# Turning the tails of two score tiles with one transpose, and regrouping the value products, in an attention and two-layer kernel

## What is computed

```python
def _attn_ref(q, k, v, tau):
    scale = 1.0 / np.sqrt(q.shape[-1])
    scores = scale * np.matmul(q, k.transpose(0, 1, 3, 2))
    thresh = np.max(scores, axis=-1, keepdims=True) - tau
    scores = np.where(scores >= thresh, scores, -1000000000.0)
    scores = scores - np.max(scores, axis=-1, keepdims=True)
    attn = np.exp(scores)
    attn = attn / (np.sum(attn, axis=-1, keepdims=True) + 1e-09)
    return np.matmul(attn, v)
# layer 1: h = x @ w_in (512 x 2048), g = h * tanh(softplus(h)), x = g @ w_out
# layer 2: h = x @ w_in, g = h * clip(h + 3, 0, 6) / 6, out = g @ w_out
```

## Time and profile before

| | |
|---|---|
| median of 3 runs | 1047.8 us (1047.51 to 1048.72) |
| the profiled execution | 1048.76 us |
| its span, first to last instruction | 1046.6 us |
| attention, first row maximum to that of the last pair | 9.0 to 300.8 us |
| PE busy over the span | 1024.9 us (98%) |
| DVE, ACT, POOL busy | 855.6, 662.0, 546.7 us |

### The profile page before, as it was taken

How to read it: one execution, slowest core, us unless ns; L and a number is a source line. 1 busy time by engine, 2 the same in 40 slices (tenths; PEclk the granted TensorE clock), 3 DMA queues, 4 the chain that set the end, 5 groups by cost and what they waited for, 6 DMA issues and landing times.

```text
span 1046.6 us, 19806 instructions
## 1 busy us (share of the span) xinstructions
PE 1024.9 (98%) x6856; PEld 920.5 (88%) x6856; DVE 855.6 (82%) x1694; ACT 662.0 (63%) x1241; POOL 546.7 (52%) x562
## 2 busy tenths in 40 slices
PE   6999999999999999999999999999999999999998
PEld 5666666666666999999999999999999999999998
DVE  7877877877773889978997889967996779968884
ACT  6778777778885566555664566646564655655643
POOL 7787887888983770078204770087103760068200
PEclk9999999999999999999999999999999999999999
DMA  6364564564542799869895899742785448843674
GB/s 189 103 215 144 161 215 143 162 215 140 177 146 82 225 327 308 321 199 294 297 371 187 266 328 315 289 142 106 250 310 163 165 164 274 281 151 127 221 242 161
DMA packets 136034, 224.37 MB, mean 214 GB/s; under 512 B 9216, under 2 KB 76288, under 8 KB 135936
## 3 DMA queue, kind: packets, MB, share of 16 engines
q1 hardware_dynamic: 135936, 223.12, 64.4%
HBM read 172.49 MB, written 50.59 MB: 213 GB/s over the span
## 4 chain that ended last, share of the span: by engine, by line
PE 79%; DVE 8%; ACT 7%; issue 4%; DMA 1%; SPq 0%; DVEq 0%; ACTq 0%
PE banks L601 8%; PE banks L548 7%; PE banks L666 7%; PE banks L668 7%; PE banks L667 7%; PE banks L703 6%; PE banks L702 6%; PE banks L701 6%; PE banks L709 5%; PE banks L711 5%; PE banks L710 5%; PE banks L560 5%; PE banks L556 3%; ACT relu L870 3%; PE banks L581 2%
## 5 line engine op out<-in xcount | busy, mean ns | idle before, releaser
L1330 POOL TENSOR_TENSOR ring<-raw,ring 128x256 fp32r<-128x256 f32 x336 | 282.3, 874 | 379.5 <-ACT ring L835 379.5
L666 PE MATMUL banks<-x_high,ring 128*128 128x384 f32 x672 | 226.7, 337 | 1.5 <-ACT probsT L774 0.8
L668 PE MATMUL banks<-x_high,ring 128*128 128x384 f32 x672 | 224.8, 334 | 0.0
L667 PE MATMUL banks<-x_low,ring 128*128 128x384 f32 x672 | 224.6, 334 | 0.0
L1010 DVE TENSOR_REDUCE neg_max<-banks 128x1 f32<-128x576 f32 x144 | 108.0, 750 | 55.6 <-PE banks L548 55.2
L703 PE MATMUL banks<-ring,g_low 128*128 128x256 f32 x504 | 142.6, 283 | 0.0
L702 PE MATMUL banks<-ring,g_high 128*128 128x256 f32 x504 | 142.6, 283 | 0.0
L701 PE MATMUL banks<-ring,g_high 128*128 128x256 f32 x504 | 142.6, 283 | 0.0
L666 PEld LDWEIGHTS banks<-x_high,ring 128*128 128x128 f32 x672 | 126.1, 188 | 7.7 <-issue 4.9
L667 PEld LDWEIGHTS banks<-x_low,ring 128*128 128x128 f32 x672 | 126.2, 188 | 0.0
L668 PEld LDWEIGHTS banks<-x_high,ring 128*128 128x128 f32 x672 | 126.1, 188 | 0.0
(11 more groups left out here) (100 smaller groups left out, 2227.7 us busy)
## 6 DMA issues: line engine op xcount, KB each, us to landing
ring<-w_out_mix SPq DMA_DIRECT2D x168, 512.0 KB, 5.0
raw<-w_in_mix SPq DMA_DIRECT2D x48, 896.0 KB, 5.9
w_in_mix<-prep_in SPq DMA_DIRECT2D x18, 896.0 KB, 5.4
w_out_mix<-prep_high SPq DMA_DIRECT2D x16, 896.0 KB, 4.7
w_out_mix<-prep_low SPq DMA_DIRECT2D x16, 896.0 KB, 5.8
q_raw<-qT SPq DMA_DIRECT2D x64, 144.0 KB, 2.9
k_raw<-kT SPq DMA_DIRECT2D x64, 144.0 KB, 2.9
prep_in<-w_in SPq DMA_DIRECT2D x64, 128.0 KB, 3.3
```

The source lines that it names most:

```text
L666: nc.tensor.matmul(dst, w[:, 0, cols], high, start=(t == 0 and m < 4), stop=False, skip_group_check=True)
L667: nc.tensor.matmul(dst, w[:, 0, cols], low, start=False, stop=False, skip_group_check=True)
L668: mm = nc.tensor.matmul(dst, w[:, 1, cols], high, start=False, stop=(t == KH - 1), skip_group_check=True)
L1330: nc.gpsimd.tensor_tensor(ring_slot(slot)[:, 1, :], raw[q % 2][:, m, :], f32(ring_slot(slot)[:, 0, :]), ALU.subtract).then_inc(w_low_ready, 1)
```

## The change

It has four parts.

1. **Tails.** The keys are put in another column order. An even tile of a pair holds keys 320 to 575, 0 to 255, and then the tail (now keys 256 to 319). An odd tile holds the tail first. The two stand next to each other in `probs`, so one 128 x 128 transpose turns both tails. Only tiles 1, 3, 5, 7 and 8 turn a tail (five per pair in place of nine), and ACT copies 128 x 128 into a new tile `tailT` (`TURNS` = 5 places). The half of the rows that belongs to the other tile meets zeros in a new tile `values_tail`, so these products have 128 rows in place of 64, and go in blocks of 128 query columns (one of 64), head after head. A tile's scores are now 320 and 256 columns, written side by side across a bank boundary. Values come in four transfers per pair in place of two.
2. **Value products** stand in four tiles (4, 6, 8, and 1 of the pair after) in place of seven. These steps turn an even tile or, at step 1, tile 8.
3. **Weight rounding** in four pieces (512, 512, 512, 256 columns), after steps 15, 16, 17 and 1. The split follows in four pieces too, and so do the late units during the layers.
4. `spread_sums` takes 128 rows everywhere.

```diff
-    PART_AT = (0, MAIN // 2 * P, SEQ)
+    X_KEYS = MAIN // 2 * P
+    Y_KEYS = X_KEYS + TAIL
+    TURNS = MAIN + 1
+    def tails_turned(t):
+        return t // PAIR_TILES * TURNS + t % PAIR_TILES // 2
+    def tail_first(i):
+        return i % 2 == 1
+    def turns_tail(i):
+        return tail_first(i) or i == PAIR_TILES - 1
+    def key_ranges(i):
+        return ((X_KEYS, SEQ), (0, X_KEYS)) if tail_first(i) else ((Y_KEYS, SEQ), (0, Y_KEYS))
...
-        scores = [banks[:, 2 * s:2 * s + 2, 0:HALF] for s in range(3)]
+        def scores_at(s):
+            first, last = key_ranges(s % PAIR_TILES)[0]
+            return BANK - (last - first)
+        def scores_of(s):
+            return bank_pair(s)[:, scores_at(s):scores_at(s) + SEQ]
+        def probs_of(t):
+            at = SEQ if tail_first(t % PAIR_TILES) else 0
+            return probs[:, tails_turned(t) % 2, at:at + SEQ]
...
-        PREP_PARTS = (slice(0, 4), slice(4, MIXES))
+        PREP_PARTS = (slice(0, 2), slice(2, 4), slice(4, 6), slice(6, MIXES))
...
-                        after(pe, tail_kept, t - 2)
+                        after(pe, tail_kept, tails_turned(max(t - 2, 0)))
...
-                nc.tensor.transpose(turned_tail[s % 3], probs[:, s % 3, SEQ - P:SEQ], ident[:, :]).then_inc(tail_turned, 1)
+                i, own = t % PAIR_TILES, probs_of(t)
+                if turns_tail(i):
+                    tail = probs[:, tails_turned(t) % 2, SEQ - TAIL:SEQ + TAIL] if tail_first(i) else own[:, SEQ - P:SEQ]
+                    nc.tensor.transpose(turned_tail[s % 3], tail, ident[:, :]).then_inc(tail_turned, 1)
...
-                    rows = slice(0 if j < MAIN else P - TAIL, P)
                     for a in range(2):
-                        mm = nc.tensor.matmul(mixed[u][DH * a:DH * a + DH, :], values[rows, b, j, DH * a:DH * a + DH],
-                                              probsT[b][rows, a, j, PART_AT[u]:PART_AT[u + 1]], start=(j == 0), stop=(j == MAIN))
+                        if j < MAIN:
+                            nc.tensor.matmul(mixed[u][DH * a:DH * a + DH, :], values[:, b, j, DH * a:DH * a + DH],
+                                             probsT[b][:, a, j, PART_AT[u]:PART_AT[u + 1]], start=(j == 0), stop=False,
+                                             skip_group_check=True)
+                            continue
+                        for c0 in range(PART_AT[u], PART_AT[u + 1], P):
+                            i = a * (MAIN + 1) + c0 // P if c0 < MAIN * P else MAIN
+                            first, n = (0, P) if i != MAIN else (TAIL * a, TAIL)
+                            rows = tail_rows(i)
+                            mm = nc.tensor.matmul(mixed[u][DH * a:DH * a + DH, c0 - PART_AT[u]:c0 - PART_AT[u] + n],
+                                                  values_tail[:, b, rows, DH * a:DH * a + DH],
+                                                  tailT[:, b, i // 2, first:first + n], start=False, stop=True, skip_group_check=True)
...
-            part0 = {4: (0,), 5: (1, 2), 6: (3, 4)}
-            part1 = {7: (0, 1), 8: (2,), 0: (3,), 1: (4,)}
+            part0 = {4: (0, 1), 6: (2, 3, 4)}
+            part1 = {8: (0, 1, 2), 1: (3, 4)}
...
-                act.wait_ge(tail_turned, t + 1)
+                if turns_tail(i):
+                    act.wait_ge(tail_turned, tails_turned(t) + 1)
+                    nc.scalar.copy(tailT[:, p, i // 2, :], turned_tail[s % 3]).then_inc(tail_kept, 1)
...
-                    if s == 16 and it < ITS - 1:
-                        round_prep(0, it, 0)
+                    if s in (15, 16, 17) and it < ITS - 1:
+                        round_prep(0, it, s - 15)
                     if s == 1 and it > 0:
-                        round_prep(0, it - 1, 1)
+                        round_prep(0, it - 1, 3)
```

More of the change, by code:

```diff
@@ L9 @@
 F32R = mybir.dt.float32r
-AX_XY = mybir.AxisListType.XY
+AX_X = mybir.AxisListType.X
 P = 128
@@ L544, in score_tile @@
                     if half == 1:
-                        after(pe, tail_kept, t - 2)
+                        after(pe, tail_kept, tails_turned(max(t - 2, 0)))
+                    first, last = key_ranges(i)[half]
+                    begin = BANK if half else scores_at(s)
                     for n, (lhs, rhs) in enumerate(products):
-                        mm = nc.tensor.matmul(scores[s % 3][:, half, :], lhs, rhs[:, HALF * half:HALF * (half + 1)],
+                        mm = nc.tensor.matmul(bank_pair(s)[:, begin:begin + last - first], lhs, rhs[:, first:last],
                                               start=(n == 0), stop=(n == len(products) - 1))
@@ L581, in spread_sums @@
                             mm = nc.tensor.matmul(mixed[u][DH * a:DH * a + DH, c0 - PART_AT[u]:c1 - PART_AT[u]],
[L582 to L583 removed]
+                                                  recips[:, b, col:col + 1].to_broadcast([P, DH]),
+                                                  ident[:, first + c0 - P * i:first + c1 - P * i], start=True, stop=True)
                 mm.then_inc(spread_ready, 1)
@@ L622, in attention_step @@
                         mix(it, pair, b, 0, part0[i])
-                    if i in (7, 8):
+                    if i == 8:
                         mix(it, pair, b, 1, part1[i])
-                if not first and i in (0, 1):
+                if not first and i == 1:
                     mix(it, pair - 1, 1 - b, 1, part1[i])
@@ L745, in round_k, with keep_main @@
                 nc.scalar.copy(k_high[k][:, :], k_raw[k % 2][:, :]).then_inc(k_high_ready[k], 1)
-            def keep_main(t, s):
+            def keep_main(t, s, pair):
                 p, i = s // PAIR_TILES, s % PAIR_TILES
                 act.wait_ge(main_turned, t + 1)
+                if i == 0:
+                    after(act, mixed_ready, 2 * pair - 2)
                 if i == MAIN:
@@ L792, in attention_step, with round_prep @@
                     after(act, probs_ready, t - 1)
-                    nc.scalar.activation(halves(exps[:, s % 2, :]), scores[s % 3], ACT.Exp,
+                    nc.scalar.activation(exps[:, s % 2, :], scores_of(s), ACT.Exp,
                                          bias=neg_max[:, s % 3:s % 3 + 1], scale=1.0).then_inc(exp_ready, 1)
                 if (not first or s >= 2) and (ahead or s < 2):
-                    keep_main(t - 2, (s - 2) % TILES_IT)
+                    keep_main(t - 2, (s - 2) % TILES_IT, it * PAIRS_IT + (s - 2) // PAIR_TILES)
                 if ahead and s in rounds:
                     round_k(it, rounds[s])
-            def round_prep(layer, u, half):
+            def round_prep(layer, u, n):
                 unit = QUADS * layer + u
@@ L939, in _ @@
                     if unit < LATE_UNITS and part == 1:
-                        for half in range(2):
-                            round_prep(*late_unit(unit), half)
+                        for n in range(len(PREP_PARTS)):
+                            round_prep(*late_unit(unit), n)
                     for b in (B22, B11, B12):
@@ L1145, in rest_prep @@
             def rest_prep(layer, u):
-                for half, mixes in enumerate(PREP_PARTS):
-                    dve.wait_ge(prep_out_rounded, 2 * (QUADS * layer + u) + half + 1)
+                for n, mixes in enumerate(PREP_PARTS):
+                    dve.wait_ge(prep_out_rounded, len(PREP_PARTS) * (QUADS * layer + u) + n + 1)
                     nc.vector.tensor_tensor(prep_low[:, mixes, :], prep_out[:, mixes, :], f32(prep_high[:, mixes, :]),
@@ L1302, in rest_prep @@
             def rest_prep(u):
-                for half, mixes in enumerate(PREP_PARTS):
-                    pool.wait_ge(prep_out_rounded, 2 * u + half + 1)
+                for n, mixes in enumerate(PREP_PARTS):
+                    pool.wait_ge(prep_out_rounded, len(PREP_PARTS) * u + n + 1)
                     nc.gpsimd.tensor_tensor(prep_low[:, mixes, :], prep_out[:, mixes, :], f32(prep_high[:, mixes, :]),
```

76 lines of the change are left out of this document (39 added, 37 removed).

## The result

| | before | after |
|---|---|---|
| median (runs) | 1047.72 us (4) | 1040.88 us (4, 1039.96 to 1042.2) |
| ratio | | 0.9936, 95% interval 0.9922 to 0.995 |
| span of the profiled execution | 1046.6 us | 1038.1 us |
| middle pair (mean of ten) | 19.61 us | 18.78 us |
| last row maximum | 318.6 us | 304.3 us |

The change makes the kernel 6.8 us faster, 0.64%. The forecast was 17.3. (The last maximum of before is at 318.6 us; the 300.8 in the table ahead is where the last pair begins.) The times between two row maxima come from the starts of that instruction, nine to a pair. The first products of the layers come in rounds of eight units, and the last row of the table is the time from the first product of a round's first unit to that of its eighth, in the second and the third round.

A forecast was written before the change was run, and what follows sets the result against it. PE's own sequence was taken to bound the attention. A gain of 1.2 us per middle pair (-12.0 for ten), smaller gains in other pairs and 0.4 given back made -17.3 us: 1030.5 us forecast, range 1026 to 1041.

The forecast's parts named there:

- The layers do not change: Layers after the attention: PE back to back, no change expected; a change above 2 us would show the prediction wrong.
- Tail transposes, -0.44: PE in attention: four tail transposes fewer per pair at 0.109 us each, -0.44 us.
- The wait behind the tail copy: Scores held behind ACT's tail copy, itself behind a rounding: 0.53 us per iteration, expected to go.
- Three groups at 0.30, -0.90: PE in attention: seven groups of value products become four, three saved at 0.30 us, -0.90 us per pair.
- Tail products, +0.06 side by side or +0.71: PE's tail products per pair: +0.06 us if both heads run at once, +0.71 us if one follows the other.
- Spread, -0.10: PE's spread of sums: 64 columns of 128 rows replace the 64-row end, -0.10 us per pair taken.
- The walk: Nine tiles stepped through three engine queues: 18.2 us per changed pair, 18.85 if heads run one after the other.
- Waits: PE's waits per pair in attention: 0.6 us before, about 0.75 us forecast after, from uneven tiles.
- DVE and ACT can't catch up: Rival, attention tiles: DVE's 1.52 us per tile holds PE, +1.9 us per pair, 1075 us; chance 0.04 (slower).
- The four-piece rounding does not do its part: Rival: POOL falls behind and delays heads, 1 to 3 us off the gain; inside the range, no separate chance.
- Heads one after the other: Rival, tail products: the second head waits for the first, 0.65 us per pair, 9 us, 1039.5 us; chance 0.33.
- No wait is left: Rival, attention: PE's work alone sets the time, -2.15 us per pair, 1018 us; chance 0.04.

The follow-up runs named there:

- e1: The changed kernel with weight rounding and splitting back in two pieces everywhere: 1035.14 us, ratio 0.9872.
- e2: The changed kernel with four rounding pieces for units rounded during the attention and two for the late units in the layers: 1035.84 us, ratio 0.9882.
- e7: The changed kernel, but in the layers ScalarE rounds in two pieces while DVE still splits in four: 1043.76 us, ratio 0.9957.
- e8: The changed kernel, but in the layers ScalarE rounds in four pieces while DVE splits in two: 1036.02 us, ratio 0.988.
- e5: The changed kernel with the value products back in seven tiles, paired tails and four-piece rounding kept: 1042.33 us, ratio 0.9941.
- e3: The changed kernel with the tail products alternating between the two heads, block by block: 1039.97 us, ratio 0.992.
- e6: The kernel before with only the value products in four tiles, each tile's tail still turned by its own transpose: 1067.48 us, ratio 1.0178.

## Why the prediction was right or wrong

**The sign and the range held** (1040.88 within 1026 to 1041), the size did not. 17.3 us were forecast and 6.8 measured. That the range held is luck: it reached so far for the rival of the heads, at 9 us, and the measured time is there by at most half of that and by a loss in the layers that had no place in the range.

**The step that failed** is the sentence "The layers do not change. Their PE is back to back, the four-piece rounding adds some 0.1 us of DVE per unit beside it". It priced the fixed cost of two more instructions, and that part is right where POOL is idle (2.15 for 2.01 us). Beside POOL each piece pays 0.54 us more: 4.27 for 2.61 us. And DVE's sums are on PE's path there. The prediction's own sign of being wrong, layers that change by more than 2 us, came true. The trace of before had it: the split stood at 2.61 us beside POOL and 2.01 without. I read durations in the attention only. The cost is 6 us of the 10.5 missing (e1, e2, e7, e8). Another 3.4 are missing in the attention, and the rest lies between one execution and the medians: the spans differ by 8.5 us, the medians by 6.8.

The Trainium skill bears on just this: the page "SBUF — State Buffer", section "Who interferes with whom", states that a DVE instruction with two SBUF inputs contends with a GpSimd instruction that reads SBUF, and that the port pair they share is an exclusive lock. The 0.54 us that each piece takes more beside POOL agree. It also names `tensor_scalar` among the operations that can take the pair, which agrees with the totals that end together with POOL's instruction.

**The attention** gave 14.3 us at the last maximum for the forecast 17.7. Term by term, per pair:

- *Tail transposes, -0.44.* Right: transposes 4.70 to 4.22 in e5, which has the old groups, and 80 tail transposes in place of 144.
- *The wait behind the tail copy.* Right: scores 7.42 to 6.90, and no score waits for a tail copy.
- *Three groups at 0.30, -0.90.* Right as PE's work, wrong as time: e5 shows the regrouping to be worth 0.02 us per pair and 1.2 us at the last maximum. The walk had put 0.75 us of waits into the changed pair, but not asked what the seven-tile pair with paired tails would wait. It waits hardly at all. The waits are the price of the four tiles, and cancel their gain.
- *Tail products, +0.06 side by side or +0.71.* Neither: products fall from 6.06 to 5.80 where 5.52 was forecast, and to 5.47 with alternating heads. So the order costs 0.32, half of the rival's 0.65. The second head passes three waiting records, not five. The rule of program order, on which the rival leant (the Trainium skill, "TensorE: Matmul & The Clock Gate", "Part 3: Packing small matmuls"), does not fit the starts measured here, if the two series are read rightly: the second head's first record starts 7 ns after the first head's first of four.
- *Spread, -0.10.* Right in size at its place and lost beside it: the 12 records at tile 3 take 0.71 in place of 0.85 (the two rows below), but the 8 at tile 2 take 0.67 in place of 0.59, and 0.85 in every second pair, where the transposes behind them wait for the main copy. In all 1.46 for 1.44.
- *Waits.* From 0.6 to some 0.87 (scores and transposes 11.53 against 10.66 of work), 0.75 forecast.

```profile
217.97 0.77 PE L626 MATMUL banks<-ident,recips 128*64 128x128 f32 x12
218.68 0.33 PE L601 MATMUL banks<-ident,probs 128*128 128x128 f32 x1
```

The pair fell by 0.83 us, where 1.2 was taken. As PE's time the heads' order (0.32) and the spread (0.10) cover the difference. That is a sum and not an experiment: with the order mended e3's pair fell by 0.13 only.

**The rivals.** "DVE and ACT can't catch up" named the right mechanism at the right tiles: light tiles that run at DVE's 1.52 us. It decides nothing on its own, for the heavy tiles make up for it. But it eats the regrouping, and in e6, with ACT at a tail copy behind each group, the same imbalance does make the kernel slower. "The four-piece rounding does not do its part" was priced at 1 to 3 us through POOL's lateness; the mechanism was another one, on DVE and in the layers. "Heads one after the other" came half true (0.32 of its 0.65 us), and its 1039.5 us lies near the measured time by coincidence. "No wait is left" did not come.

## What to carry to other kernels

An instruction that is cut into pieces pays its waits once per piece. Before splitting a DVE operation with two SBUF inputs, compare its duration beside a running GpSimd instruction and alone, in every stage that calls the same helper. And when a regrouping is to save TensorE time, walk the arrangement without it too, after the other edits: here its 0.87 us per pair were just the waits that it brought, and without the regrouping e5 had 13.1 of the attention's 14.3 us.

## What was not expected of the hardware

- Some DVE instructions take turns with POOL's, one by one: the subtraction of two SBUF tiles went from 0.68 us alone to 1.22, and an addition of a constant on 9 columns, 0.17 us long, took up to 1.69 us (e3). The reciprocal of the same 9 columns took 0.21 us in the middle of a POOL instruction.
- On the two column halves of TensorE, the second head's records, as I read the two series, start past three waiting records of the first. With six in front they started only at the first head's third, and the group cost 0.27 us more than in the alternating order (0.92 and 0.65).
- The same edit, alternating the heads, was worth 0.13 us per pair with the totals and four pieces, and 0.29 without the totals and with two. Which of the two made the difference is open.
